# Moving an identity matrix and five small statistics buffers behind the large SBUF buffers of a fused attention and two-MLP kernel

## The reference, cut to what matters

```python
qn = q / (norm(q, axis=1) + 1e-06)          # q, k, v: (1, 6016, 256)
kn = k / (norm(k, axis=1) + 1e-06)
s = kn.transpose(0, 2, 1) @ qn / tau        # 256 x 256
a = softmax(s)
x = v @ a
g = x @ w_gate                              # 256 -> 1536
y = (g * sigmoid(g) * (x @ w_val)) @ w_out  # -> 256
h = y @ w_in2                               # 256 -> 2048
out = (h * clip(h + 3, 0, 6) / 6) @ w_out2  # -> 256
```

## Time and profile before

| | before |
|---|---|
| three runs | 1199.22, 1200.28, 1200.36 us |
| median | 1200.28 us |
| profiled execution, span from first to last instruction | 1197.2 us (its own run time is not listed) |
| PE busy | 1182.3 us, 99% |
| DVE, ACT, POOL busy | 719.6, 287.3, 80.1 us |
| mean granted TensorE clock | 0.997 |

### The profile page before, as it was taken

One profiled execution on the slowest core, in us unless ns is written; L12 is line 12 of the kernel. 1 busy time (PEld: TensorE's weight loads), 2 busy tenths in 40 slices (PEclk: granted clock), 3 DMA queues, 4 the chain that ended last, 5 costly groups with the idle time before them and its releaser, 6 DMA issues.

```text
span 1197.2 us, 14739 instructions
## 1 busy us (share of the span) xinstructions
PE 1182.3 (99%) x5274; PEld 975.8 (82%) x5274; DVE 719.6 (60%) x1162; ACT 287.3 (24%) x456; POOL 80.1 (7%) x47
## 2 busy tenths in 40 slices
PE   8899999999999999999999999999999999999998
PEld 7788888888888888888888888888888888888998
DVE  5788664665574475485476466466457447547555
ACT  7541221221122121122122122122212212112121
POOL 5775000000000000000000000000000000000000
PEclk9899999999999999999999999999999999999999
DMA  9733010002002002002002001000200200100100
GB/s 340 231 95 82 1 26 10 0 2 33 0 0 35 0 0 35 0 0 35 0 0 35 0 0 22 13 0 0 35 0 0 35 0 0 31 0 0 18 2 14
DMA packets 108111, 33.76 MB, mean 28 GB/s; under 512 B 98624, under 2 KB 102464, under 8 KB 108096
## 3 DMA queue, kind: packets, MB, share of 16 engines
q1 hardware_dynamic: 107952, 33.56, 11.7%
q10 hardware_dynamic: 144, 0.00, 0.0%
HBM read 27.39 MB, written 6.16 MB: 28 GB/s over the span
## 4 chain that ended last, share of the span: by engine, by line
PE 97%; issue 1%; DVE 1%; POOL 0%; ACT 0%; POOLq 0%; DVEq 0%; ACTq 0%
PE psum L691 33%; PE psum L668 32%; PE psum L679 22%; PE psum L703 6%; PE psum L568 3%; PE psum L653 1%; PE psum L563 0%; DVE diag_q L456 0%; POOL qk_parts L299 0%; DVE norms L450 0%; PE psum L612 0%; DVE act_out L523 0%; PE psum L622 0%; DVE prod L510 0%; PE psum L616 0%
## 5 line engine op out<-in xcount | busy, mean ns | idle before, releaser
L691 PE MATMUL psum<-prod,down_w 128*128 128x512 f32 (+1 forms) x1728 | 439.0, 392 | 0.0
L691 PEld LDWEIGHTS psum<-prod,down_w 128*128 128x128 f32 x1728 | 324.0, 188 | 70.3
L679 PE MATMUL psum<-yT,up_w 128*128 128x512 f32 (+1 forms) x1152 | 289.5, 392 | 0.0
L679 PEld LDWEIGHTS psum<-yT,up_w 128*128 128x128 f32 x1152 | 216.0, 189 | 48.3
L523 DVE TENSOR_TENSOR act_out<-psum,act_out 128x512 f32<-128x512 f32 (+1 forms) x144 | 97.9, 680 | 245.3 <-PE psum L668 214.4
L668 PE MATMUL psum<-vT,gate_w 128*128 128x512 f32 (+1 forms) x864 | 218.7, 388 | 0.1
L668 PE MATMUL psum<-vT,val_w 128*128 128x512 f32 (+1 forms) x864 | 216.6, 386 | 0.0
L668 PEld LDWEIGHTS psum<-vT,gate_w 128*128 128x128 f32 x864 | 161.5, 188 | 35.4 <-DVE act_out L523 0.9
L668 PEld LDWEIGHTS psum<-vT,val_w 128*128 128x128 f32 x864 | 161.5, 188 | 33.1
L536 DVE SCALAR_TENSOR_TENSOR act_out<-act_out,psum 128x512 f32<-128x512 f32 (+1 forms) x192 | 129.3, 673 | 89.7 <-ACT act_out L395 89.6
L387 ACT ACTIVATE act_out<-psum 128x512 f32<-128x512 f32 (+1 forms) x144 | 84.9, 589 | 402.6 <-PE psum L668 378.8
(11 more groups left out here) (68 smaller groups left out, 354.7 us busy)
## 6 DMA issues: line engine op xcount, KB each, us to landing
qk<-in_q SPq DMA_DIRECT2D x11, 512.0 KB, 4.9
qk<-in_k SPq DMA_DIRECT2D x11, 512.0 KB, 6.2
v_in<-in_v SPq DMA_DIRECT2D x44, 128.0 KB, 3.4
out<-out_sb SPq DMA_DIRECT2D x44, 128.0 KB, 3.0
w_stage<-in_moe_w_out SPq DMA_DIRECT2D x7, 512.0 KB, 3.8
w_stage<-in_moe_w_in SPq DMA_DIRECT2D x4, 512.0 KB, 3.8
raw_up<-in_moe_w_gate SPq DMA_DIRECT2D x3, 512.0 KB, 6.9
raw_up<-in_moe_w_val SPq DMA_DIRECT2D x3, 512.0 KB, 7.7
```

What stands on the lines that cost most here:

```text
L679: end = mm(HID[j % 4][:, 0:n], up2_w[:, part, b, j * P:(j + 1) * P], yT[:, m, b, 0:n], start=(part, m, b) == (0, 0, 0), stop=(part, m, b) ...
L691: end = mm(banks[h][:, 0:n], w[:, part, j, h * P:(h + 1) * P], prod[:, c % 4, m, 0:n], start=j == 0 and (part, m) == PASSES[0], stop=False)
```

## The change

Six calls of `sb` move from ahead of the second `early` stack to behind `act_out`. No instruction, semaphore, order or shape changes; the addresses above do. All lines below the move come two lines earlier in the changed file (L691 becomes L689).

```diff
         expT = sb("expT", [P, 2, KC, C], fp32r)
-        ident = sb("ident", [P, P])
-        tau_sb = sb("tau_sb", [P, 1])
-        neg_scale = sb("neg_scale", [P, KC])
-        neg_max = sb("neg_max", [P, KC])
-        row_sum = sb("row_sum", [P, KC])
-        row_rec = sb("row_rec", [P, KC])
-
-
         with ExitStack() as early:
             qk_first = sb("qk_first", [P, 2, FIRST * C], fp32, early)
...
         yT = sb("yT", [P, 2, KC, BANK], fp32r)
         out_sb = sb("out_sb", [P, BANK // SQUARE * KC, SQUARE])
         act_out = sb("act_out", [P, 2, BANK])
+        ident = sb("ident", [P, P])
+        tau_sb = sb("tau_sb", [P, 1])
+        neg_scale = sb("neg_scale", [P, KC])
+        neg_max = sb("neg_max", [P, KC])
+        row_sum = sb("row_sum", [P, KC])
+        row_rec = sb("row_rec", [P, KC])
```

## The result

The changed kernel takes **1173.51 us** (median of 4 runs, 1173.08 to 1173.75) beside 1200.26 us for the kernel before; the ratio is 0.9777, 95% interval 0.9763 to 0.9791. That is 26.8 us less; forecast was 1174.0, range 1171 to 1184.

What follows compares the result with a forecast made beforehand. TensorE, busy 1182.3 of 1197.2 us, was taken as the bound. Savings of 26.1 us in full tiles and 0.3 us in the last bring the span to 1170.8 us; adding 3.1 us gives 1174 us, range 1171 to 1184.

Steps and rivals of the forecast that it cites:

- The pace: Full tiles: all 408 matmuls at 226.7 ns, so a tile falls from 94.86 to 92.49 us; -26.1 us over eleven tiles.
- The last tile: Final tile with 384 columns: 72 matmuls gain 3.4 ns each, plus a little at the first ones of `up2`; -0.3 us.
- The prologue: Stretch before the first tile: moved `ident` and statistics cost the same, 0, with +-2.4 us kept for DVE operations shifting against GpSimd.
- From span to run time: Whole kernel: the median of runs stands 3.1 us above the profiled span, turning 1170.8 us into 1174 us.
- The hand-over: Between the two MLPs: slack before the first reader of `yT`'s low part shrinks from 0.37 to 0.31 us, no wait.
- the slower rival: Between the MLPs: DVE and ACT operations grow, costing 3.2 us over 12 tiles while TensorE gains nothing; 1203.5 us, chance 0.04.
- The 32 bytes are not the cause: Matmuls on `prod` and `yT`: the pace belongs to something that stays, so no difference, 1200.3 us; chance 0.09.
- yT alone: Second MLP: `yT` matmuls gain 7.5 ns, those on `prod` nothing; 7.9 us saved, 1192.4 us, chance 0.05.
- The rule on 16 byte lines: SBUF reads: 2048 bytes cover the same 128 lines from either start, so no gain, 1200.3 us; no chance of its own.

## Why the prediction was right, and where it was not

**The pace.** Term: 264 matmuls a tile on `prod` and `yT` go from 234.2 to vT's 226.7 ns, the tile from 94.86 to 92.49 us. Measured: 92.48. Eleven tiles give 26.2 us where I had 26.1. The comparison of L668 with L679 at equal shape carried the forecast.

**The last tile.** -0.3 us was forecast, and the part from its first matmul to the end went from 76.8 to 76.4 us (starts at 1120.34 and 1095.22 us).

**The prologue.** 0 with a bound of 2.4 us. In the two profiles the first tile begins at 76.4 and 77.5 us. With a gap of 672 bytes, where all large buffers lie as before, it is 77.5 too; but there the small tensors have moved as well. The kernel with the other order of `up2`, whose small tensors have not, has 76.8, and so has the one with the weights moved, whose have. The two kinds overlap, so no term of the change shows; spread between executions is the likely reason.

**From span to run time.** I took over the 3.1 us by which the median stood above the span before. In the changed kernel it stands only 1173.51 - 1171.6 = 1.9 us above, while the span came out 0.8 us over the forecast 1170.8. The two nearly cancel, so it is in part luck that the time was met to 0.5 us.

**The hand-over.** 0.31 us of slack forecast, 0.30 found, no wait in full tiles. In the last one the 24 matmuls of L677 take 4.25 us where 24 x 173.3 ns are 4.16, the few tens of nanoseconds that I had allowed for, and some more. DVE's low part of `yT` takes 0.69 us in both kernels, so the slower rival had no ground.

**The step that failed** is the reading of the cause. I ruled weight loads out because "every weight tensor begins at a multiple of 128 bytes in both files". That excludes that the weights changed, not that the moving operand is good or bad only against them. `vT` was fast not because it stood at a multiple of 128, but because it stood where the weights stand, modulo 256; the diff happened to bring `prod` and `yT` to that place. Had it brought them to a multiple of 256, which satisfies the same description, my argument would have said 1174, and the kernel takes 1193.98. The range was right by the luck of one residue.

**The rivals.** "The 32 bytes are not the cause" fell with the gap of 672 bytes, and its support from the last tile with the other order of `up2`. My answer to it, that 384 columns have slack, was wrong for that kernel: the slack came with a wait. It would hold at distances of 32 and 64. Its other support was that `qk_first` ran no slower than `qk`. The kernel's L568 takes both operands from one buffer, at offsets that are multiples of 512 bytes, so their distance modulo 256 is 0 wherever the buffer lies; this never spoke against the distance. No run here moved them apart. "yT alone" fell with `prod` alone moved. The rule on 16 byte lines foretold no gain; measured is 26.8 us.

**Open.** Why the distance matters is not shown. The rows of a matmul and of a weight load start some 3 ns apart in the second MLP of all these traces. A clash between reading the two operands is a natural guess; it is argued only. Why 64 is better than 32, 96 and 128, and why short waits end the slow state with 384 columns at a distance of 160 but not at 96 or 128, is open. In full tiles of the kernel before no such wait was seen, so whether one would end it there is untested. `vT` and the first MLP's weights were not moved by themselves, and shifts of both to other places than 32 were not tried. No kernel here beats the changed one.

## What to carry to other kernels

Compare the distance between matmul starts of equal shape but different operands: a few nanoseconds on each of thousands are a per cent of a TensorE-bound kernel, and no wait shows them. Then look at the start addresses of the moving operand and of its weights together, modulo 256, and bring them to the same residue, which was the best place here for float32r with 512 columns; a few bytes of small tensors allocated ahead of large ones are enough to lose it. And test "aligned" with a second aligned place before believing it.

## What the runs showed of the hardware that was not expected

- With 512 columns, 128 x 128 weights and a fresh weight load for each float32r matmul, the pace is 226.7 ns when moving operand and weights have the same residue modulo 256, 228.8 ns at a distance of 64, 233.3 to 234.3 ns at 32, 96, 128, 160 and 224, and 237.5 ns at 4 (239.3 with yT at 132 in turn).
- The slow pace outlasts its cause a little: the vT groups behind a prod group took 1.40 and 1.37 us; at the head of a tile, where more vT groups follow, the third is back at 1.36.
- With 384 columns and a distance of 160 the slow pace is 176.7 ns against 173.3, and two starts late by some 20 ns ended it for the rest of the kernel; without them it stayed. At distances of 32 and 64 prod ran at 173 ns from its first groups in the last tile.
